# Half of the attention scores streamed over 64 columns: exchanged key halves, three transposes, and a new order of loads

## The chip, the cores and the metric

The kernel runs on one core of a Trainium2 chip. The metric is the device time of one execution, in microseconds. Before the change it was 646.65 us, the median of three runs (646.60, 646.65 and 646.69).

## What is computed

The reference chains three layers. A linear attention with a decay per channel and a bonus for the current token comes first, over 2 batches, 8 heads, 768 tokens and 48 channels per head. Its output, 1536 tokens of 384 features, goes through a feed-forward layer with ELU (384 to 2048 to 384) and then through four dense experts with ReLU (384 to 1024 to 384), weighted by normalised probabilities.

```python
def _attn_ref(r, k, v, w, u):
    for t in range(S):
        cur = np.einsum('bhd,bhe->bhde', u[None] * kt, vt)
        y[:, :, t] = np.einsum('bhd,bhde->bhe', rt, state + cur)
        state = wt[:, :, :, None] * state + np.einsum('bhd,bhe->bhde', kt, vt)

x = attn_out.transpose(0, 2, 1, 3).reshape(1536, 384)
h = x @ w_in
x = np.where(h > 0, h, np.exp(np.minimum(h, 0)) - 1) @ w_out
p = domain_probs / (domain_probs.sum(-1, keepdims=True) + 1e-9)
out = sum(p[:, e:e+1] * (np.maximum(x @ w1[e], 0) @ w2[e]) for e in range(4))
```

## The kernel before

The 1536 tokens are 12 chunks of 128 (6 per batch, the batches taken in turn), numbered 0 to 11. In a chunk, tokens are held in the order 63 down to 0, then 64 to 127: the first half is turned round, and decays are taken from the middle of the chunk. Heads go in four pairs `p`; of a pair, head `o` = 0 lies in partitions 0 to 47 and head `o` = 1 in 64 to 111.

For each chunk the attention does this. VectorE forms running products of the decays (`products`, `inverses`), scales k and r with them (`scale_k` L892, `scale_r` L906), and TensorE multiplies them to scores, keys by queries (`scores`, L1183 to 1202). GpSimd puts the bonus on the diagonal of `att` (`bonus_terms` L519 to 528, `bonus_diagonal` L531 to 538), VectorE copies the scores over it where the mask allows (`mask_scores` L909 to 922), and TensorE multiplies with the old state (`old_values` L1279) and with v (`values_even` L1291, `values_odd` L1295 and L1299). For the state, k has to be turned: VectorE transposes it in blocks of 32 x 32 (`turn_blocks` L895 to 900), SP writes the blocks to DRAM and reads them back as `kt_sb` (`move_blocks`, L455 and L460), and TensorE multiplies them with v (`update`, L1233). Chunks 0 and 1 go another way (scores at L1196, turned on TensorE); chunks 2 to 9 are turned as said, and 10 and 11, the last of each batch, need no update.

Scores of keys in the second half (64 to 127) and queries in the first (0 to 63) are always masked. Before the change they are computed all the same: for each pair and head two matmuls, one for each half of the keys, each over all 128 queries. A matmul of fp32 is two records in the trace. With 48 rows and 64 columns of weights the four (o, half) of a pair lie in four quadrants of the array.

The attention doesn't run by itself. TensorE's order is written out by hand as steps `n` of the first feed-forward layer: a step is an up-projection of one slice of 128 hidden features for one tile of tokens, and a down-projection of the step but one before (`LAG` = 2). Tiles have 256, 256, 512 and 512 tokens, 16 slices each. `SCORES` says in which step a chunk's scores stand: chunk c at 4c up to 8, then every third step, at the end of the step; its values follow two steps later. Other operations have their step relative to that (`PRODUCTS` -4, `HALF_INVERSES` -3, `SCALE_K` -2, `SCALE_R` -1, turned k in the step of `scale_k`, but for chunks 3, 4 and 8 one later, behind `scale_r`: `LATE_TURNS`). VectorE and ScalarE serve the feed-forward layer in the same queues. ScalarE takes relu and exp of the hidden values (L763, L765), VectorE finishes the ELU in PSUM (L997), ScalarE rounds it (`hi_g` L771), VectorE takes the rest (`lo_g` L1003), since every product is made in three passes of high and low parts.

Weights are split likewise: in the first tile ScalarE copies each slice rounded to `w_hi` (L723 and L728, in halves from slice 6, where `HI_BETWEEN` says: slice 12 in step 9, 13 in 10, 14 in 11, 15 in 12 and 13), and GpSimd (`lo_w` L547) or VectorE (L967) takes the rest to `w_lo`. GpSimd's queue is w_lo halves, with the bonus terms of chunks 2 and 3 and their diagonals between.

All loads here are on SP's queue, in the order of its program: decays and k, r of chunks 0 and 1, constants, v of 0 and 1, slices 0 to 7, `load_rkw(2)`, `load_tok(2)`, u, slices 8 and 9, `load_rkw(3)`, `load_tok(3)`, slices 10 to 15, probabilities; then for c = 4 to 11 `load_rkw(c)` (k, r and decays by channel, L442), `load_tok(c)` (r, k and v by token, L449) and `move_blocks(c - 2)`. `load_rkw(c)` waits for the values of chunk c-3, `move_blocks` for the turned blocks, its reads also for the landing of its write. Three buffers each hold the chunks in turn.

After 165 us only the feed-forward layers run. The change doesn't touch them.

## Time and profile before

| | |
|---|---|
| median of 3 runs | 646.65 us (646.60 to 646.69) |
| the profiled execution | 646.8 us |
| its span | 645.0 us |
| instructions | 13796 |
| TensorE matmul busy | 638.5 us (99%) |
| TensorE weight load busy | 591.7 us (92%) |
| VectorE busy | 419.4 us (65%) |
| ScalarE busy | 237.2 us (37%) |
| GpSimd busy | 296.1 us (46%) |

The profile is one execution. Its time of 646.8 us lies 0.15 us above the median, and 1.8 us of it lie around the span. Times in the trace count from the span's start. PE is TensorE's matmuls, PEld its weight loads, DVE VectorE, ACT ScalarE, POOL GpSimd, SPq the DMA issues of SP. A row of the timeline merges neighbours of one kind: start, time from the first start to the last end, line, operation, what it writes and reads, how many. In brackets stands the idle time in front of it and what ended it. Matmuls overlap in the array, so the distance from start to start is what one costs, not its duration.

### The profile page before, as it was taken

The page shows a single profiled execution, that of the slowest core. Times are in us where ns is not written, and L with a number is a line of the kernel's source. Part 1 is how long each engine was busy: PE and PEld are TensorE (multiplying, and loading weights), DVE is VectorE, ACT ScalarE, POOL GpSimd, SP SyncE. Part 2 cuts the span into 40 slices and gives each one's busy share as a digit, 9 for nine tenths or more (in the row PEclk, how much of TensorE's full clock was granted, in tenths as well). Part 3 has the DMA queues.
Part 4 walks back from the last instruction along what each step waited for, and adds up shares of the span by engine and source line. Part 5 has one row for each costly group of instructions (what it writes and reads, how often), then busy time and mean ns, then how long its engine had stood idle before and what let it go on. Part 6 is the DMA issues. An engine that isn't in the chain of part 4 may idle for free.

```text
span 645.0 us, 13796 instructions
## 1 busy us (share of the span) xinstructions
PE 638.5 (99%) x5046; PEld 591.7 (92%) x5046; DVE 419.4 (65%) x786; ACT 237.2 (37%) x557; POOL 296.1 (46%) x370
## 2 busy tenths in 40 slices
PE   8999999999999999999999999999999999999998
PEld 5998999877788888999999999999999999999997
DVE  7889999874357666565555555565656565656564
ACT  4785555655445554222222222222222222222221
POOL 5897424420799899994029900019900018000000
PEclk9999999999999999999999999999999999999999
DMA  9954454300000233000013100012100011001011
GB/s 328 404 186 137 138 182 162 124 14 1 1 2 1 73 98 100 27 2 0 1 50 99 50 1 0 1 49 99 50 1 0 0 50 50 0 1 49 0 50 50
DMA packets 19043, 42.34 MB, mean 66 GB/s; under 512 B 2608, under 2 KB 8752, under 8 KB 18992
## 3 DMA queue, kind: packets, MB, share of 16 engines
q1 hardware_dynamic: 18704, 41.23, 18.7%
q8 instruction: 36, 0.59, 0.4%
q10 hardware_dynamic: 288, 0.39, 0.2%
q14 instruction: 15, 0.12, 0.1%
HBM read 37.16 MB, written 4.46 MB: 65 GB/s over the span
## 4 chain that ended last, share of the span: by engine, by line
PE 91%; DVE 3%; POOL 3%; issue 1%; DMA 0%; ACT 0%; DVEq 0%; POOLq 0%
PE bank L1366 29%; PE bank L1367 29%; PE bank L1368 29%; POOL w_lo L547 3%; PE bank L1200 1%; PE bank L1279 1%; PE bank L1291 1%; DVE fr L864 1%; DMA rkw<-rkw_dram 0%; DVE fr L883 0%; PE bank L1233 0%; PE bank L1299 0%; PE bank L1295 0%; DVE w_lo L967 0%; DVE rkw L906 0%
## 5 line engine op out<-in xcount | busy, mean ns | idle before, releaser
L1366 PE MATMUL bank<-x_lo,w_hi 128*128 128x256 f32 (+2 forms) x416 | 138.0, 332 | 0.6 <-POOL w_lo L547 0.5
L1367 PE MATMUL bank<-x_hi,w_lo 128*128 128x256 f32 (+2 forms) x416 | 135.2, 325 | 0.0
L1368 PE MATMUL bank<-x_hi,w_hi 128*128 128x256 f32 (+2 forms) x416 | 135.2, 325 | 0.0
L1367 PE MATMUL bank<-w_hi,g_lo 128*128 128x384 f32 x384 | 129.6, 337 | 0.0
L1368 PE MATMUL bank<-w_hi,g_hi 128*128 128x384 f32 x384 | 129.3, 337 | 0.0
L1366 PE MATMUL bank<-w_lo,g_hi 128*128 128x384 f32 x384 | 129.0, 336 | 0.0
L827 ACT ACTIVATE g_hi<-bank 128x512 fp32r<-128x512 f32 x96 | 57.5, 599 | 144.3 <-DVE bank L1053 122.4
L1366 PEld LDWEIGHTS bank<-x_lo,w_hi 128*128 128x128 f32 x416 | 78.2, 188 | 10.4 <-issue 2.5
L1368 PEld LDWEIGHTS bank<-x_hi,w_hi 128*128 128x128 f32 x416 | 78.2, 188 | 7.5
L1367 PEld LDWEIGHTS bank<-x_hi,w_lo 128*128 128x128 f32 x416 | 78.3, 188 | 7.1
L1046 DVE TENSOR_TENSOR u_sum<-p_copy,bank 128x256 f32<-128x256 f32 x56 | 23.6, 421 | 92.1 <-ACT p_copy L751 91.3
L559 POOL TENSOR_TENSOR raw<-raw 128x128 f32<-128x128 f32 x16 | 7.5, 469 | 160.5 <-DMA raw<-w_dram 160.5
L1366 PEld LDWEIGHTS bank<-w_lo,g_hi 128*128 128x128 f32 x384 | 72.2, 188 | 0.0
L1368 PEld LDWEIGHTS bank<-w_hi,g_hi 128*128 128x128 f32 x384 | 72.1, 188 | 0.0
L1367 PEld LDWEIGHTS bank<-w_hi,g_lo 128*128 128x128 f32 x384 | 72.0, 188 | 0.0
L1135 DVE SCALAR_TENSOR_TENSOR g_lo<-bank,g_hi 128x512 fp32r<-128x512 f32 x96 | 65.9, 686 | 7.1 <-ACT g_hi L827 6.8
L751 ACT COPY p_copy<-bank 128x256 f32<-128x256 f32 x56 | 21.0, 375 | 134.4 <-PE bank L1368 134.2
L1366 PE MATMUL bank<-g_lo,w_hi 128*128 128x256 f32 (+1 forms) x192 | 65.1, 339 | 0.0
L1368 PE MATMUL bank<-g_hi,w_hi 128*128 128x256 f32 (+1 forms) x192 | 64.9, 338 | 0.0
L1367 PE MATMUL bank<-g_hi,w_lo 128*128 128x256 f32 (+1 forms) x192 | 64.7, 337 | 0.0
L571 POOL TENSOR_TENSOR w_lo<-raw,w_hi 128x768 fp32r<-128x768 f32 x32 | 58.6, 1855 | 0.0
L1051 DVE TENSOR_TENSOR bank<-p_copy,bank 128x256 f32<-128x256 f32 x56 | 24.0, 429 | 51.4 <-PE bank L1368 51.4
(134 smaller groups left out, 1272.6 us busy)
## 6 DMA issues: line engine op xcount, KB each, us to landing
raw<-w_dram SPq DMA_DIRECT2D x48, 384.0 KB, 3.7
rkw<-rkw_dram SPq DMA_DIRECT2D x10, 772.5 KB, 4.6
tok<-tok_dram SPq DMA_DIRECT2D x10, 576.0 KB, 6.8
k_blocks_dram<-k_blocks SPq DMA_DIRECT2D x8, 256.0 KB, 4.3
kt_sb<-k_blocks_dram SPq DMA_DIRECT2D x32, 64.0 KB, 2.0
out_dram<-acc SPq DMA_DIRECT2D x10, 192.0 KB, 1.9
rkw<-rkw_dram SPq DMA_DIRECT2D x2, 512.0 KB, 4.2
rkw<-rkw_dram SPq DMA_DIRECT2D x2, 260.5 KB, 3.4
```

Source lines behind the costliest of these rows:

```text
L547: pool.tensor_tensor(w_lo[:, n, part], raw[:, n, part], w_hi[:, n, part].bitcast(F32), ALU.subtract).then_inc(s_wq, 1)
L559: pool.tensor_tensor(s1, a21, a22, ALU.add).then_inc(s_ws, 1)
L571: pool.tensor_tensor(w_lo[:, slot, :], raw[:, slot, :], w_hi[:, slot, :].bitcast(F32), ALU.subtract).then_inc(s_w, 1)
L751: act.copy(p_copy[:, 0, :], bank[6][:, 0:QUARTER]).then_inc(s_pc, 1)
L827: act.activation(g2[0][:, p % 2 * 2 + o, :], bank[o][:, :], ACT.Relu).then_inc(s_gh, 1)
L864: dve.tensor_tensor_scan(fr[:, 0:SCAN], rkw[c % DEEP][:, 2 * NRK:2 * NRK + SCAN], reset[:, :], 0.0, ALU.mult, ALU.add).then_inc(s_f, 1)
L1046: dve.tensor_tensor(u2, p1, p6, ALU.add).then_inc(s_u2, 1)
L1051: dve.tensor_tensor(c11, p1, c11, ALU.add).then_inc(s_c, 1)
L1135: dve.scalar_tensor_tensor(out=g2[1][:, r, :], in0=bank[o][:, :], scalar=0.0, in1=g2[0][:, r, :].bitcast(F32), op0=ALU.max, op1=ALU.subtra ...
L1366: pe.matmul(out, wh, ml, start=start, stop=False, skip_group_check=shared)
L1367: pe.matmul(out, wl, mh, start=False, stop=False, skip_group_check=shared)
L1368: return pe.matmul(out, wh, mh, start=False, stop=stop, skip_group_check=shared)
```

## The change

- `scores`, chunks 2 to 11: of each head, the matmul of the early keys streams all 128 queries, that of the late keys only the 64 late ones. For pairs 0 and 1 (`exchanged`) the late keys are written to partitions 0 to 63 of the bank and the early ones to 64 to 127; for pairs 2 and 3 as before. The order goes by two pairs, 0 and 2, then 1 and 3, and the pairs lie in the bank as 0, 2, 1, 3 (`place`). Still 16 matmuls.
- All that meets the exchanged keys follows. By-token rows of heads 0 to 3 are loaded with halves exchanged: `load_tok` is three DMAs (64 rows, 64 rows, 128 rows, each of 3 x 192 columns) and not one. Turned k: `turn_blocks` is three transposes of 128, 128 and 256 columns. The diagonal is three selects of 256, 256 and 512 elements, not two of 512. A second mask with exchanged halves is loaded by two small DMAs behind `load_tok(3)`, and `mask_scores` uses both masks, on two blocks of 256 columns. It waits for all three selects where the first half waited for one, and in chunk 2 for the mask. The sums of the bonus are written in another order of heads.
- `move_blocks` becomes `write_blocks` and `read_blocks`, and both stand ahead of `load_tok`. Slices 12 and 13 stand between the write and the reads of chunk 2, slices 14 and 15 behind `load_tok(4)`.

```diff
             def load_rkw(c):
                 need(sp, s_py, c - DEEP + 1)
-                need(sp, s_kb, c - DEEP + 1 - FIRST)
+                need(sp, s_kb, 3 * (c - DEEP + 1 - FIRST))
...
-                sp.dma_start(tok[c % DEEP][:, :], tok_d[c]).then_inc(s_tok[c % DEEP], 16)
...
+                sp.dma_start(columns(here[0:HALF, :], 0), columns(there[HALF:CH, :], 0)).then_inc(s_tok[c % DEEP], 16)
+                sp.dma_start(columns(here[HALF:CH, :], 0), columns(there[0:HALF, :], 0)).then_inc(s_tok[c % DEEP], 16)
+                sp.dma_start(columns(here[:, :], DM // 2), columns(there, DM // 2)).then_inc(s_tok[c % DEEP], 16)
...
-            sp.dma_start(const[:, :], const_d).then_inc(s_const, 16)
+            sp.dma_start(const[:, P:3 * P], const_d[:, C_MASK:C_MASK + 2 * P]).then_inc(s_const, 16)
...
-            load_slices(10, 11, 12, 13, 14, 15)
+            for rows, others in ((slice(0, HALF), slice(HALF, CH)), (slice(HALF, CH), slice(0, HALF))):
+                sp.dma_start(const[rows, 0:P], const_d[others, C_MASK:C_MASK + P]).then_inc(s_exchanged, 16)
+            load_slices(10, 11)
             sp.dma_start(probs[:, :, :], probs_d).then_inc(s_probs, 16)
             for c in range(4, NC):
                 load_rkw(c)
+                write_blocks(c - 2)
+                if c == 4:
+                    load_slices(12, 13)
+                read_blocks(c - 2)
                 load_tok(c)
-                move_blocks(c - 2)
+                if c == 4:
+                    load_slices(14, 15)
...
-                for o in range(2):
-                    pool.affine_select(att[:, o, :, :], heads[:, o, :].unsqueeze(2).broadcast_to([P, PAIRS, CH]),
...
+                diagonal(0, 0, HALF, HALF)
+                diagonal(0, HALF, HALF, 0)
+                diagonal(1, 0, CH, 0)
...
-                dve.transpose(k_blocks[:, :, :].rearrange("q t (a j) -> q t a j", a=PAIRS),
-                              raw_k(c).rearrange("q (a t i) -> q t a i", a=PAIRS, i=STRIP)).then_inc(s_kb, 1)
+                strips = raw_k(c).rearrange("q (a t i) -> q t a i", a=PAIRS, i=STRIP)
+                turned = k_blocks[:, :, :].rearrange("q t (a j) -> q t a j", a=PAIRS)
+                dve.transpose(turned[:, 0:2, 0:2, :], strips[:, 2:4, 0:2, :]).then_inc(s_kb, 1)
+                dve.transpose(turned[:, 2:4, 0:2, :], strips[:, 0:2, 0:2, :]).then_inc(s_kb, 1)
+                dve.transpose(turned[:, :, 2:4, :], strips[:, :, 2:4, :]).then_inc(s_kb, 1)
...
-                    dve.wait_ge(s_diag, diagonal_done(c) - 1 + o)
-                    dve.copy_predicated(att[:, o, :, :], masks.bitcast(I32), found).then_inc(s_att, 1)
+                    dve.wait_ge(s_diag, diagonal_done(c))
+                    found = banks["x"][o][:, :].rearrange("p (a t) -> p a t", a=PAIRS // 2)
+                    dve.copy_predicated(att[:, o, :, :].rearrange("p (a b) t -> p a (b t)", b=2),
+                                        both_masks.unsqueeze(1).broadcast_to([P, PAIRS // 2, 2 * CH]).bitcast(I32),
+                                        found).then_inc(s_att, 1)
...
+                def block(p, o, later, first, count):
+
+                    rows, at = slice(64 * o, 64 * o + D), HALF * (later != exchanged(p))
+                    out = place(c, p) * CH + first
+                    return pe.matmul(banks["x"][o][at:at + HALF, out:out + count],
+                                     k[rows, p * CH + HALF * later:p * CH + HALF * later + HALF],
+                                     q[rows, p * CH + first:p * CH + first + count], start=True, stop=True)
+
+                for p in range(PAIRS // 2):
+                    for one in (p, p + PAIRS // 2):
+                        for o in range(2):
+                            block(one, o, 0, 0, CH)
+                        for o in range(2):
+                            ins = block(one, o, 1, HALF, HALF)
```

## Rows read from the trace of the kernel before

**Rows 1.** The page: TensorE's busy time, and the chain by engine.
```profile
PE 638.5 (99%) x5046; PEld 591.7 (92%) x5046; DVE 419.4 (65%) x786; ACT 237.2 (37%) x557; POOL 296.1 (46%) x370
...
PE 91%; DVE 3%; POOL 3%; issue 1%; DMA 0%; ACT 0%; DVEq 0%; POOLq 0%
```

**Rows 2.** Timeline of TensorE at two waits: start, time, line, what, [idle before <-releaser].
```profile
37.21 0.36 PE L1366 MATMUL bank<-x_lo,w_hi 128*128 128x256 f32 x1 [0.51 <-POOL w_lo L547]
...
61.45 0.34 PE L1200 MATMUL bank<-rkw 48*64 48x128 f32 x4 [0.44 <-DVE rkw L906]
```

**Rows 3.** Windows by stage: length, busy time by engine, granted clock, DMA share, GB/s.
```profile
17.00:37.00 20.00, 19.70 (x218) 18.95 (x213) 17.67 (x39) 15.82 (x45) 18.15 (x23) 1.00 0.96 376
...
61.00:73.50 12.50, 12.03 (x193) 11.46 (x192) 11.80 (x25) 7.16 (x24) 4.39 (x6) 1.00 0.47 160
```

**Rows 4.** Timeline of VectorE: turned k of chunk 5, scaled r of chunks 5, 6, 7.
```profile
70.97 0.71 DVE L899 STREAM_TRANSPOSE k_blocks<-rkw 128x512 f32<-128x512 f32 x1
71.60 0.70 DVE L931 TENSOR_TENSOR st<-bank,st 64x192 f32<-64x192 f32 x2
...
72.80 0.69 DVE L906 TENSOR_TENSOR rkw<-rkw,fr 128x512 f32<-128x512 f32 x1
...
84.53 0.69 DVE L906 TENSOR_TENSOR rkw<-rkw,fr 128x512 f32<-128x512 f32 x1
...
96.27 0.69 DVE L906 TENSOR_TENSOR rkw<-rkw,fr 128x512 f32<-128x512 f32 x1
```

**Rows 5.** Timeline of TensorE: the first scores of chunks 5, 6 and 7.
```profile
73.55 0.34 PE L1200 MATMUL bank<-rkw 48*64 48x128 f32 x4
...
85.49 0.34 PE L1200 MATMUL bank<-rkw 48*64 48x128 f32 x4
...
97.44 0.34 PE L1200 MATMUL bank<-rkw 48*64 48x128 f32 x4
```

**Rows 6.** Timeline of ScalarE: its waits on TensorE in chunks 7 and 8.
```profile
94.35 0.39 ACT L763 ACTIVATE neg<-bank 128x256 f32<-128x256 f32 x1 [0.68 <-PE bank L1368]
...
106.31 0.39 ACT L763 ACTIVATE neg<-bank 128x256 f32<-128x256 f32 x1 [0.90 <-PE bank L1368]
```

**Rows 7.** Timeline of TensorE: tiled matmuls, and what follows the scores of chunk 8.
```profile
16.46 0.67 PE L1225 MATMUL bank<-tok,kt_sb 128*64 128x48 f32 x16
...
104.49 0.52 PE L1233 MATMUL bank<-tok,kt_sb 128*32 128x48 f32 x32
...
110.40 1.10 PE L1200 MATMUL bank<-rkw 48*64 48x128 f32 x32
...
111.43 0.50 PE L1366 MATMUL bank<-x_lo,w_hi 128*128 128x512 f32 x1
```

**Rows 8.** VectorE by line and form, 61 to 97 us: busy, mean ns | idle before.
```profile
L1003 DVE TENSOR_TENSOR g_lo<-bank,g_hi 128x256 fp32r<-128x256 f32 x13 | 5.3, 409 | 1.3 <-ACT g_hi L771 1.3
...
L950 DVE TENSOR_TENSOR x_lo<-bank,x_hi 128x384 fp32r<-128x384 f32 x2 | 1.1, 549 | 0.0
...
L873 DVE RECIPROCAL inv_end<-fr 128x8 f32<-128x8 f32 x3 | 0.6, 207 | 0.1
```

**Rows 9.** Timeline of GpSimd and VectorE: diagonal and mask of chunk 5.
```profile
74.83 1.22 POOL L536 TENSOR_SCALAR_AFFINE_SELECT att<-bonus_sb 128x512 f32<-128x512 f32 x2 [7.59 <-DVE bonus_sb L938]
...
77.87 1.36 DVE L922 COPY_PREDICATED att<-const,bank 128x512 f32<-128x512 int32 x2
```

**Rows 10.** Timeline of SP and ScalarE, the landings of L455, DMA issues of slices.
```profile
32.74 0.33 SPq L455 DMA_DIRECT2D k_blocks_dram<-k_blocks  x1
37.39 1.86 SPq L460 DMA_DIRECT2D kt_sb<-k_blocks_dram  x4
...
45.74 0.91 ACT L728 CAST w_hi<-raw 128x384 fp32r<-128x384 f32 x2
...
DMA to landing us min/median/max: 2.0/4.3/5.8
...
raw<-w_dram SPq DMA_DIRECT2D x48, 384.0 KB, 3.7
```

More of the change, by code:

```diff
@@ L295, in bass_linear_attention_elu_ffn_dense_experts, with tok_landed, exchanged, place @@
         s_dr = sem("s_dr")
-        mask = const[:, C_MASK:C_MASK + P]
-        ident = const[:, C_ID:C_ID + P]
+        both_masks = const[:, 0:2 * P]
+        mask = const[:, P:2 * P]
+        ident = const[:, 2 * P:3 * P]
         def landed(eng, sems, c):
             eng.wait_ge(sems[c % DEEP], 16 * (c // DEEP + 1))
+        def tok_landed(eng, c):
+            parts = 3 * (c // DEEP + 1) - (2 if c % DEEP < FIRST else 0)
+            eng.wait_ge(s_tok[c % DEEP], 16 * parts)
+        def exchanged(p):
+            return p < PAIRS // 2
+        def place(c, p):
+            return p if c < FIRST else p % 2 * 2 + p // 2
         def raw_q(c):
@@ L937, in bonus @@
                 bonus_done(dve, c - 2)
-                dve.tensor_reduce(bonus_sb[:, c % 2, :], tok[c % DEEP][:, 0:DM].rearrange("p (h d) -> p h d", h=H),
+                dve.tensor_reduce(bonus_sb[:, c % 2, :].rearrange("p (b o a) -> p b a o", b=2, o=2),
+                                  tok[c % DEEP][:, 0:DM].rearrange("p (b a o d) -> p b a o d", b=2, o=2, d=D),
                                   AX.X, ALU.add).then_inc(s_bon, 1)
```

63 lines of the change are left out of this document (35 added, 28 removed).

## The prediction

> **What bounds the kernel now.** I read the shares of busy time first: TensorE is busy 99% of a 645.0 us span, and the chain that ended last is 91% TensorE [rows 1]. From the windows view on, the question is therefore not whether TensorE bounds the whole, but where another engine sets its pace for a while, since only the attention part (17 to 165 us) is touched. The view of waits sent me to two such places in TensorE's timeline: at 37.21 us, 0.51 us on GpSimd's `w_lo` (slice 9), and at 61.45 us, 0.44 us on the vector engine's scaled r in front of the scores of chunk 4 [rows 2]. The windows by stage show why the second matters: from 61 to 73.5 us VectorE is busy 11.80 of 12.50 us, nearly as full as TensorE, while DMA is at 0.47; from 17 to 37 us it is DMA that is full, 0.96; the granted clock is 1.00 in both [rows 3].
>
> Next I set the ends of the scaled r beside the starts of the scores that need it. Chunk 5: r ends at 72.80+0.69 = 73.49, scores start at 73.55. Chunk 6: 85.22 and 85.49. Chunk 7: 96.96 and 97.44 [rows 4, 5]. The handover takes some 0.06 us (chunk 5, where TensorE had waited), so the slack is 0, 0.21, 0.42 us. VectorE goes round in 11.73 us per chunk (72.80, 84.53, 96.27), TensorE in 11.94 and 11.95. That VectorE isn't carried along by TensorE in this stretch, the scalar engine shows: its one wait on TensorE per chunk grows from 0.68 to 0.90 us [rows 6], which it would not if both went at one pace. So from about 46 us (where I place the start, after the GpSimd wait at 37 and the update of chunk 2) to 97 us there are two loops side by side, VectorE with ScalarE at 11.73 and TensorE at 11.95 us per chunk, and VectorE's lead at the end is 0.42 us. Behind that, with tiles of 512 tokens, TensorE alone is the bound.
>
> **The scores.** One chunk has 16 matmuls, 32 records, in four quadrants of the array. From the row, starts are (1.10-0.27)/31 = 26.8 ns apart, or 107 ns per pass of 128 columns in one quadrant; from the first score to the next matmul of another line it is 111.43-110.40 = 1.03 us [rows 7]. Eight passes per quadrant make 0.86 us of it. The change leaves the number of matmuls, but half of them stream 64 columns, and since the halves of pairs 0 and 1 are exchanged each quadrant gets four long and four short passes. Nothing before has a 64-column pass. From below: half of 107, 53 ns. From above, no gain at all, 107 ns. The nearest row is that of L1225, weights of 64 columns as here and 48 columns streamed: (0.67-0.22)/15 = 30 ns for two tiles, 60 ns per pass; with weights of 32 columns the same 48 take (0.52-0.21)/31 x4 = 40 ns [rows 7]. So the load of 64 weight columns, not the stream, seems to set some 58 to 60 ns. I take 58: 4 x (107-58) = 0.20 us saved per chunk. All of it on TensorE is 10 x 0.20 = 2.0 us. Whether four quadrants really work independently when the passes are unequal is open; if matmuls start strictly in order, a short pass can wait behind a long one of another quadrant, and counting out the order loses 0.05 us a chunk. That is kept in the range.
>
> The Trainium skill, page "TensorE: Matmul & The Clock Gate", section "Wait — 56ns, not 53.3ns?", says that starts of matmuls are never closer than about 25 ns, however few columns they have. The 26.8 ns of the row are just above that, and by the rule this edit would save at most 32 x 1.8 ns a chunk. The trace doesn't agree for matmuls in separate tiles: L1233 starts one every (0.52-0.21)/31 = 10 ns [rows 7]. The case is a rival below all the same.
>
> **VectorE.** `turn_blocks` becomes three transposes of 128, 128 and 256 columns for one of 512. The elements are the same, so two fixed costs come on top. Operations of 256 and 384 columns take 409 and 549 ns, so 128 columns are 0.14 us; a transpose of 512 is followed 71.60-70.97 = 0.63 us later, and 0.63-4x0.14 leaves 0.07 fixed [rows 4, 8]. From below: 0 (hidden in its neighbours, or in a wait). From above: the 207 ns that an operation of 8 columns takes from start to end [rows 8], if the parts don't overlap at all. I take 0.10 each, since the row of 0.07 is the nearest and a wait or a semaphore may add a little: d = 0.20 us per turn. In the queue of VectorE, the turn of chunk 3 stands before the scaled r of chunk 4, that of chunk 4 before the r of chunk 5, and those of 5, 6 and 7 before their own: five turns in the self-paced stretch. (The turn of chunk 2 lies ahead of the GpSimd wait, those of 8 and 9 where TensorE is the bound.) There, VectorE falls back by 5 x 0.20 = 1.0 us.
>
> The Trainium skill, page "VectorE: DVE Perf Modes", section "The TRN2 errata", speaks against this split too: each operation pays a fixed cost, 58 cycles for a source in SBUF. As an estimate from that page it is 2 x 0.06 = 0.12 us a turn and 0.6 us for five turns instead of 1.0.
>
> `mask_scores` reads the same 512 columns twice; it now waits for all diagonals before the first half. Behind it in the queue stand an ELU and the factors of the next chunk, and the values of the chunk wait for it. But GpSimd's diagonal ends at 74.83+1.22 = 76.05, a third instruction adds 0.1, and the mask starts at 77.87 [rows 9]: nothing. The reduction writes its 8 sums in another order, same elements: nothing. The extra wait for the exchanged mask falls on chunk 2 only, with its load issued in the first 20 us.
>
> **Queues.** By-token loads become three DMAs, two more issues of about 0.5 us on SP each for chunks 2 to 11, in pieces of 768 bytes. From chunk 4 on they stand behind the moves of turned k, used a chunk later by GpSimd: nothing on the path. In front they cost SP 1 us twice before slices 8 and 10, while DMA is a full queue anyhow [rows 3]. Then SP's order is: write of chunk 2 (after its turn, 32.74 now), slices 12 and 13, four reads, tok 4, slices 14 and 15. The reads were issued at 37.39, 4.6 us behind the write; such a write lands in 2.0 us at best and 5.8 at worst [rows 10], and with four slices of 384 KB gone from the full stretch I take 2.0. Then, at some 0.47 us an issue, as the four reads show, and 3.7 us from issue to landing for a slice [rows 10]: slices 12 and 13 at 33.9 + 3.7 = 37.6; reads issued by 35.2 + 1.9 = 37.1, tok 4 by 38.5, slices 14 and 15 at 39.4 + 3.7 = 43.1. If the write again takes 4.6 us, this is 45.7. ScalarE copies slice 14 at 45.74 [rows 10], and 12 and 13 one and two steps ahead of that. So the cover is 2.6 us, and hardly any at the bad end; if it went, the scalar engine's queue would stop, with its `g_hi` copies behind, and VectorE with it. For later chunks turned k no longer stands behind tok in the DMA queues, which gives its update more slack; no update waits for it now, so nothing is gained.
>
> GpSimd gets one more select in front of `w_lo` halves 9 to 12, 0.1 us; the wait at 37.21 lies before it. That wait takes the saving of chunk 2's scores whole, since TensorE then only waits longer.
>
> **The sum.** Scores of chunk 7 start when VectorE delivers: 96.96+0.06+1.0 = 98.02, against 97.44 now, +0.58 us. The savings of chunks 2 to 6 are all spent in waits there. From chunk 7 on TensorE is the bound again: five chunks (7 to 11) save 5 x 0.20 = 1.0. Together -0.42 us. Against the profiled execution (645.0 us span, 646.8 in all) that is 646.4; the median of the runs is 646.65, and from there I forecast **646.2 us**. In terms of d the change is -1.42 + 5d: at d = 0 it gives 645.2, at the upper bound, 0.40, 647.2.
>
> **The rivals.**
> - TensorE takes the full gain (12%): the two added transposes hide in VectorE's waits on the scalar engine (some 0.9 us per chunk, 12.50-11.80 and the like [rows 3]). Chunks 4 to 11 save 8 x 0.20: -1.6, 645.0. Against it: those waits are answers to VectorE's own ELU and move with it.
> - The short matmuls gain nothing (8%), be it by a floor on starts or because the weight load holds each quadrant. The scores stay at 1.03 us, only the loss of VectorE stays: +0.58, 647.2. Against it: matmuls in separate tiles start 10 ns apart, and the 48-column passes of L1225 take 60 ns, not 107 [rows 7]. (The Trainium skill's 25 ns between starts, cited above, would be such a floor.)
> - Slower (8%): slices 14 and 15 behind the by-token load come late. The copy of slice 14 stands at 45.74 in ScalarE's queue, and from there to 97 us each late microsecond passes to VectorE and on to the scores. With the forecast's -0.4 it makes the kernel slower at all from a landing at 46.2 us, and measurably from 47.5; at 48.2 it gives 646.2 + 2.4 = 648.6. For it: three DMAs with six times as many pieces, and a step that waits for the turn. Against: 2.6 us of cover.
> - The order makes no difference that counts (2%): the compiled quadrants behave as before and the turns cost nothing, 646.6.
>
> **Chances.** The forecast's case has 70%: its own range, with d from 0 to 0.40, is 645.2 to 647.2, and 0.05 us a chunk less on the scores adds 0.25. The range 645.2 to 647.3 takes in the floor rival as well and leaves out the full gain, 0.2 below it, and the late slices. About 0.2%, 1.3 us, is what a measurement of this kernel can tell from no change. Faster than 645.35 is the full gain and a small part of my own case: 0.16. Slower than 647.95: 0.08. The same: 0.76.
>
> **What would show it.** Right: scores of a chunk take 0.83 us from first to next line; TensorE waits on scaled r at the scores of chunks 4 to 7, in all over 1 us; chunk 7's scores start near 98.0; chunk 11's near 150.7. Wrong: no such waits (the turns are free), an unchanged 1.03 us for the scores, or ScalarE waiting on a weight slice between 39 and 50 us. The prediction falls with d above all: each 0.1 us of it is worth 0.5 us.

## The result: 648.49 us, slower by 0.3%, and the profile after

The changed kernel takes 648.49 us in the median of 9 runs (648.34 to 649.29), the kernel before 646.60 us (646.55 to 646.75, 9 runs). The ratio is 1.0031, 95% interval 1.0022 to 1.0039: slower, by 1.9 us. The forecast was 646.2 us and the range ended at 647.3. The profiled execution is the slowest of the nine, 649.29 us with a span of 647.6 us, 0.8 above the median; against the span before, 645.0, it shows 2.6 us to be explained. The difference between the medians is 1.9 us; no execution near the median was traced, so the waits below may be up to 0.8 us longer than in a typical one.

The line numbers have moved: scores L1200 are L1251, passes of the steps L1366 to L1368 are L1425 to L1427, scaled r L906 is L947, turned k L899 is L939 to L941, ScalarE's copy of a slice L728 is L766. From the page of the changed kernel, busy time and chain (as [rows 1]):

```profile
PE 637.0 (98%) x5046; PEld 590.2 (91%) x5046; DVE 421.3 (65%) x802; ACT 237.0 (37%) x557; POOL 296.7 (46%) x380
...
PE 81%; DVE 9%; SPq 3%; ACT 3%; issue 2%; DMA 1%; POOL 0%; DVEq 0%; ACTq 0%; POOLq 0%
```

TensorE had 91% of the chain and has 81%. SP and DMA, with nothing to speak of before, now hold 4% of it, and the windows view says where. Its columns are those of [rows 3]; the last two are the DMA share and the rate in GB/s.

```profile
17.00:37.00 20.00, 17.83 (x172) 17.09 (x173) 16.00 (x36) 12.85 (x35) 16.50 (x23) 1.00 0.89 274
61.00:73.50 12.50, 11.70 (x189) 10.90 (x188) 11.84 (x26) 7.27 (x25) 6.88 (x11) 1.00 0.36 115
```

From 17 to 37 us TensorE does 17.83 us of work instead of 19.70, and DMA moves 274 GB/s instead of 376. The timelines of ScalarE, then of TensorE, in that stretch:

```profile
32.33 0.51 ACT L766 CAST w_hi<-raw 128x384 fp32r<-128x384 f32 x1 [2.74 <-DMA raw<-w_dram]
```
```profile
33.63 0.39 PE L1425 MATMUL bank<-g_lo,w_hi 128*128 128x256 f32 x1 [1.36 <-DVE g_lo L1050]
...
36.83 0.39 PE L1425 MATMUL bank<-g_lo,w_hi 128*128 128x256 f32 x1 [0.81 <-DVE g_lo L1050]
...
38.09 0.90 PE L1251 MATMUL bank<-rkw 48*64 48x128 f32 x32
...
38.92 0.39 PE L1425 MATMUL bank<-x_lo,w_hi 128*128 128x256 f32 x1
```

ScalarE stands 2.74 us for weight slice 10. Its `g_hi` stands behind the copy in its queue, VectorE's `g_lo` waits for that, and TensorE for `g_lo`: 1.36 and 0.81 us. The scores of chunk 2 start at 38.09 us; before, they started at 35.60. The chain that ended last, from 19 us on, names what made the slice late:

```profile
19.41 2.39 SPq L515
...
21.84 0.79 SPq L515
...
22.67 9.64 DMA raw<-w_dram
...
32.33 0.02 ACT w_hi L766
```

And SP's own timeline ahead of that:

```profile
13.71 3.00 SPq L444 DMA_DIRECT2D raw<-w_dram  x2
16.75 0.43 SPq L457 DMA_DIRECT2D rkw<-rkw_dram  x1
17.36 0.70 SPq L468 DMA_DIRECT2D tok<-tok_dram  x1
18.11 0.61 SPq L469 DMA_DIRECT2D tok<-tok_dram  x1
18.76 0.61 SPq L470 DMA_DIRECT2D tok<-tok_dram  x1
19.41 3.22 SPq L515 DMA_DIRECT2D const<-const_dram  x2
22.67 1.93 SPq L444 DMA_DIRECT2D raw<-w_dram  x2
```

In the kernel before, SP and ScalarE had this:

```profile
10.59 0.93 SPq L429 DMA_DIRECT2D raw<-w_dram  x2
...
17.59 2.81 SPq L429 DMA_DIRECT2D raw<-w_dram  x6
```
```profile
29.72 0.50 ACT L728 CAST w_hi<-raw 128x384 fp32r<-128x384 f32 x1
```

SP issues the two small mask loads for 3.22 us, slices 8 and 9 for 3.00 and slices 10 and 11 for 1.93 us, where two slices took 0.93 us before: it is held up. Slices 8 and 9 are issued 3.1 us later than before, slice 10 5.1 us later, at 22.67 and not at 17.59. By the landings slice 10 arrives at 32.31 us, before at 28.52, where its copy began at 29.72. So there were 1.2 us of cover (the time between the landing of a transfer and its first use), and the delay was 3.8.

The delay stays. Starts of the scores in us, chunks 2 to 11 (first L1200 or L1251 of each, from TensorE's timeline):

```
chunk      2      3      4      5      6      7       8       9      10      11
before  35.60  48.08  61.45  73.55  85.49  97.44  110.40  125.35  141.35  150.96
after   38.09  50.49  63.96  76.45  88.47 100.48  113.25  128.58  144.38  153.79
later    2.49   2.41   2.51   2.90   2.98   3.04    2.85    3.23    3.03    2.83
```

2.4 to 2.5 us are lost before chunk 3. All that the new scores save (ten times 0.20 us) is spent again. A step that kept its saving would be 0.20 us shorter than before. From chunk 4 to 5 it is 0.39 us longer (12.49 against 12.10), from 8 to 9 0.38 (15.33 against 14.95), and from 5 to 6 and 6 to 7 it takes 12.02 us instead of 11.95; from 7 to 8 and behind 9 the saving is there.

### The profile page after: what moved, and what is told of

It is laid out like the page before. It is cut to its first block, busy times and chain, and to the rows that moved or that the text cites. A ratio compares the mean times of both kernels' runs of the same rounds, so it can differ in the third digit from the quotient of the medians.

```text
span 647.6 us, 13845 instructions
## 1 busy us (share of the span) xinstructions
PE 637.0 (98%) x5046; PEld 590.2 (91%) x5046; DVE 421.3 (65%) x802; ACT 237.0 (37%) x557; POOL 296.7 (46%) x380
## 4 chain that ended last, share of the span: by engine, by line
PE 81%; DVE 9%; SPq 3%; ACT 3%; issue 2%; DMA 1%; POOL 0%; DVEq 0%; ACTq 0%; POOLq 0%
PE bank L1425 27%; PE bank L1426 26%; PE bank L1427 26%; DVE bank L1044 2%; DVE fr L902 2%; DMA raw<-w_dram 1%; DVE att L966 1%; SPq L444 1%; DVE rkw L930 1%; ACT neg L801 1%; ACT neg L803 1%; ACT alpha L728 1%; ACT g_hi L809 1%; DVE fr L921 1%; DVE st L977 0%
## 5 line engine op out<-in xcount | busy, mean ns | idle before, releaser
L1425 PE MATMUL bank<-x_lo,w_hi 128*128 128x256 f32 (+2 forms) x416 | 138.1, 332 | 0.5 <-POOL w_lo L585 0.4
L1427 PE MATMUL bank<-x_hi,w_hi 128*128 128x256 f32 (+2 forms) x416 | 135.2, 325 | 0.0
L1427 PE MATMUL bank<-w_hi,g_hi 128*128 128x384 f32 x384 | 129.3, 337 | 0.0
L1425 PE MATMUL bank<-w_lo,g_hi 128*128 128x384 f32 x384 | 129.0, 336 | 0.0
L1425 PEld LDWEIGHTS bank<-x_lo,w_hi 128*128 128x128 f32 x416 | 78.2, 188 | 9.6 <-issue 1.0
L1427 PEld LDWEIGHTS bank<-x_hi,w_hi 128*128 128x128 f32 x416 | 78.2, 188 | 7.5
L1425 PEld LDWEIGHTS bank<-w_lo,g_hi 128*128 128x128 f32 x384 | 72.1, 188 | 0.0
L1427 PEld LDWEIGHTS bank<-w_hi,g_hi 128*128 128x128 f32 x384 | 72.0, 188 | 0.0
L1425 PE MATMUL bank<-g_lo,w_hi 128*128 128x256 f32 (+1 forms) x192 | 65.5, 341 | 2.8 <-DVE g_lo L1050 2.2
L1427 PE MATMUL bank<-g_hi,w_hi 128*128 128x256 f32 (+1 forms) x192 | 64.9, 338 | 0.0
L609 POOL TENSOR_TENSOR w_lo<-raw,w_hi 128x768 fp32r<-128x768 f32 x32 | 58.5, 1852 | 0.0
```

Source lines behind the costliest of these rows:

```text
L609: pool.tensor_tensor(w_lo[:, slot, :], raw[:, slot, :], w_hi[:, slot, :].bitcast(F32), ALU.subtract).then_inc(s_w, 1)
L1425: pe.matmul(out, wh, ml, start=start, stop=False, skip_group_check=shared)
L1427: return pe.matmul(out, wh, mh, start=False, stop=stop, skip_group_check=shared)
```

## The experiments

Two questions: what held up slice 10, and where the saved 2 us went. Every kernel ran beside the kernel before on the same chip. Given are the median and the ratio to the kernel before with its 95% interval.

### Slices 10 and 11 first

```diff
             load_slices(8, 9)
+            load_slices(10, 11)
             load_rkw(3)
             load_tok(3)
...
-            load_slices(10, 11)
             sp.dma_start(probs[:, :, :], probs_d).then_inc(s_probs, 16)
```

> The changed kernel with one thing altered: weight slices 10 and 11 are issued ahead of chunk 3's loads instead of behind them and the two small mask DMAs. Theory A (the time was lost because slice 10 landed 3.8 us later than before, behind by-token loads cut into 768-byte pieces, so that ScalarE stood 2.74 us for it): slice 10 lands near 28.5 us again, ScalarE's wait of 2.74 us for it goes, the scores of chunk 2 start near 35.7 instead of 38.1, and the time falls by 1.9 to 2.4 us, to 646.2 to 646.8. Rival B (the time was lost in the chunks, on VectorE: two more transposes in each turn of k and a scan that lasts 0.14 us longer): the first chunks come earlier but the end hardly does, 648.0 to 648.5. Rival C (chunk 3's loads now arrive late instead): a wait of ScalarE or GpSimd for chunk 3's tok of 1 us or more, 647.5 to 648.5.

646.76 us, ratio to the kernel before 1.0003 (0.9994 to 1.0012). ScalarE's timeline again:

```profile
29.62 0.50 ACT L766 CAST w_hi<-raw 128x384 fp32r<-128x384 f32 x1
```

The wait is gone, chunk 2's scores start at 35.51. One line moved gives back 1.7 us, and the kernel can't be told from the one before. The load by token of chunk 3 now lands at 32.3 us instead of 31.1, and GpSimd wants it at 47 only: rival C is out. Rival B is out as the cause of the loss, but what it describes is there: from chunk 5 on its scores start 0.35 to 0.8 us behind those of the kernel before.

### The pieces alone

In the kernel before, a load by token as three DMAs, for which all its readers wait:

```diff
-                sp.dma_start(tok[c % DEEP][:, :], tok_d[c]).then_inc(s_tok[c % DEEP], 16)
+                sp.dma_start(columns(here[0:HALF, :], 0), columns(there[0:HALF, :], 0)).then_inc(s_tok[c % DEEP], 16)
+                sp.dma_start(columns(here[HALF:CH, :], 0), columns(there[HALF:CH, :], 0)).then_inc(s_tok[c % DEEP], 16)
+                sp.dma_start(columns(here[:, :], DM // 2), columns(there, DM // 2)).then_inc(s_tok[c % DEEP], 16)
```

> The kernel before with one part of the change alone: each load by token goes as three DMAs with 768-byte pieces for r and k's first and second halves of the columns, with nothing exchanged, and those who read it wait for all three. The order of all loads is that of before, slices 10 to 15 follow chunk 3's loads, and the two small mask DMAs are not there. Theory A (the 768-byte pieces hold up the slices): slice 10 lands 3 to 4 us later than before (31.5 to 32.5 instead of 28.52), ScalarE waits for it, and the kernel is 1.8 to 2.5 us slower than before, 648.4 to 649.1. If the mask DMAs carry half of it, slice 10 lands near 30.5 and the time is 647.2 to 647.8. Rival B (VectorE in the chunks): 646.5 to 646.8, since no work of VectorE is added here.

650.56 us (649.10 to 656.78), ratio 1.0072 (1.0044 to 1.0100). With no mask load and nothing exchanged, slice 10 lands at 31.9 us, 3.4 of the 3.8 us late. ScalarE waits 1.37 us for it, and chunk 2's scores start at 37.10, 1.5 us late where the changed kernel had 2.5. The rest of the 3.9 us comes later and is more than I gave the pieces: in the order of before, in which turned k stands behind the loads by token, TensorE's update of chunk 2 comes to wait as well (and another, for 0.6 us, between the scores of chunks 6 and 7):

```profile
46.03 0.55 PE L1244 MATMUL bank<-tok,kt_sb 128*32 128x48 f32 x32 [1.71 <-DMA kt_sb<-k_blocks_dram]
```

The changed kernel, with the same pieces and the new order of the moves, has no such wait.

### Pieces twice as large

In the kernel before, three DMAs again, but r, k and v whole:

```diff
-                sp.dma_start(tok[c % DEEP][:, :], tok_d[c]).then_inc(s_tok[c % DEEP], 16)
+                for i in range(3):
+                    part = slice(i * DM, (i + 1) * DM)
+                    sp.dma_start(tok[c % DEEP][:, part], tok_d[c][:, part]).then_inc(s_tok[c % DEEP], 16)
```

> The kernel before with each load by token as three DMAs of r, k and v whole: as many DMAs and issues on SP as in the changed kernel, but pieces of 1536 bytes instead of 768. Theory (the small pieces fill the queues): a third of the way or less, slice 10 lands by 29.5 us, ScalarE waits less than 0.3 us for it, and the time is 646.5 to 647.0. Rival (three issues on SP for one and their share of the queue, whatever the pieces): slice 10 lands at 31 us or later and the time is that of the kernel with the 768-byte pieces, above 648.

647.14 us, 1.0005 (0.9996 to 1.0014), 0.3 us over the 646.85 of its group. Slice 10 lands at 28.5 us, as before, and is copied at 29.66. There are as many DMAs for a load as in the change, and nothing is lost for the slices: it isn't their number but their form. The form differs in two ways, though. The pieces are of 1536 bytes and not of 768, and all three DMAs cover 128 rows, where two of the change's three cover 64. No run separates these two. In the changed kernel the DMA records of chunk 3's 768-byte pieces, in the order of their start, have medians of 45 and 72 ns for the two quarters that should be the DMAs of 64 rows and of 54 and 46 for those of the third, so the pieces are dear in both; which piece belongs to which DMA the records don't tell. The windows view from 18 to 30 us, where DMA is full, for the kernel before, the changed kernel, the pieces alone, and this one:

```profile
18.00:30.00 12.00, 12.00 (x129) 11.68 (x128) 10.42 (x23) 9.10 (x25) 10.59 (x14) 1.00 1.02 401
```
```profile
18.00:30.00 12.00, 12.00 (x129) 11.67 (x128) 10.44 (x24) 8.90 (x24) 10.59 (x14) 1.00 1.07 300
```
```profile
18.00:30.00 12.00, 11.98 (x128) 11.58 (x127) 10.42 (x22) 8.47 (x23) 10.45 (x15) 1.00 1.07 318
```
```profile
18.00:30.00 12.00, 12.00 (x128) 11.68 (x128) 10.42 (x23) 9.15 (x25) 10.59 (x14) 1.00 1.04 392
```

The share is over 1 in all four: by it the changed kernel's DMA is as full as ever, but it moves 300 GB/s instead of 401. Over 12 us that is 1.2 MB less, or 3.0 us at the old rate, most of the 3.8 us by which slice 10 is late. With 1536-byte pieces it is 392.

### The halves exchanged in DRAM

```diff
-                sp.dma_start(columns(here[0:HALF, :], 0), columns(there[HALF:CH, :], 0)).then_inc(s_tok[c % DEEP], 16)
-                sp.dma_start(columns(here[HALF:CH, :], 0), columns(there[0:HALF, :], 0)).then_inc(s_tok[c % DEEP], 16)
-                sp.dma_start(columns(here[:, :], DM // 2), columns(there, DM // 2)).then_inc(s_tok[c % DEEP], 16)
+                sp.dma_start(tok[c % DEEP][:, :], tok_d[c]).then_inc(s_tok[c % DEEP], 16)
...
+    tok[FIRST:, :, :, 0:DM // 2] = np.roll(tok[FIRST:, :, :, 0:DM // 2], HALF, axis=1)
```

> The changed kernel with r and k by token already exchanged in DRAM for the late chunks, so that a load by token is one DMA in pieces of 4608 bytes again; the order of all loads, with slices 10 and 11 behind chunk 3's loads and the mask DMAs, is that of the changed kernel. Theory A (the pieces, not the place of slice 10): slice 10 lands near 29 us, ScalarE's wait of 2.74 us is gone, and the time is that of the run with the slices first, 646.5 to 646.9. Rival (the two mask DMAs and the order are at fault, and the run with the slices first only stepped around them): slice 10 lands at 30.5 us or later, ScalarE waits 0.8 us or more for it, and the time is 647.3 to 648.5.

646.87 us, 1.0002 (0.9993 to 1.0011): as with the slices first. Slice 10 lands at 28.5, the copy starts at 29.70, though the mask loads and the order are those of the change. SP issues the two mask loads in 1.19 us here instead of 3.22:

```profile
17.58 1.19 SPq L508 DMA_DIRECT2D const<-const_dram  x2
```

They are slow only where the queues hold the small pieces. The mask loads and the order don't cost this time by themselves.

### The order alone

The kernel before with turned k in front of the loads by token, slices 12 and 13 behind its write, 14 and 15 behind tok 4.

```diff
                 load_rkw(c)
+                write_blocks(c - 2)
+                if c == 4:
+                    load_slices(12, 13)
+                read_blocks(c - 2)
                 load_tok(c)
-                move_blocks(c - 2)
+                if c == 4:
+                    load_slices(14, 15)
```

> The kernel before with the new order of SP's queue alone: turned k is moved in front of the loads by token, slices 12 and 13 behind its write, 14 and 15 behind tok 4. By the prediction nothing is won or lost: slice 14 lands near 43 us, copied near 45.7, and the time is 646.5 to 646.8. If the slices come late (46.2 us or later), up to 648.6. If turned k's earlier arrival is worth something, under 646.4.

646.71 us, 1.0000 (0.9991 to 1.0009). Slice 14 lands at 42.6 us, where the prediction worked out 43.1. That is near by luck in part: it was issued at 36.94 and not at 39.4, and took 5.6 us and not 3.7.

### The scores alone

In the kernel before, with `block` as in the change but the pairs in their old places. The masks, the diagonal, turned k and the by-token loads stay unexchanged, so for pairs 0 and 1 this kernel leaves out what would make its result the attention; it only measures the time.

```diff
-                        for half in range(2):
-                            keys = slice(p * CH + HALF * half, p * CH + HALF * half + HALF)
-                            ins = pe.matmul(banks["x"][o][HALF * half:HALF * half + HALF, cols], k[rows, keys],
-                                            q[rows, cols], start=True, stop=True)
...
+                for p in range(PAIRS // 2):
+                    for one in (p, p + PAIRS // 2):
+                        for o in range(2):
+                            block(one, o, 0, 0, CH)
+                        for o in range(2):
+                            ins = block(one, o, 1, HALF, HALF)
```

> The kernel before with the new scores alone, in the late chunks: two pairs write their key halves to exchanged partitions, and the masked quarter is not computed. Everything behind it (mask, diagonal, k turned, r and k by token) stays unexchanged, so what it computes for these two pairs is not the attention of the reference; the work on all engines but TensorE is that of before. It measures the saving where VectorE keeps its old load. By the prediction's formula with no added turn cost: -1.42 us, 645.2, scores of chunk 7 at 97.0 and TensorE waiting for scaled r there. If VectorE's own pace is slower than the 11.73 us that I read (it may have been carried along by TensorE), less: -1.0, 645.6. If it is TensorE that paces all ten chunks: -2.0, 644.6.

645.65 us, 0.9985 (0.9977 to 0.9994): faster, by 1.05 us. The scores take 0.83 us. TensorE's timeline, chunks 5 to 8:

```profile
73.45 0.90 PE L1204 MATMUL bank<-rkw 48*64 48x128 f32 x32
...
85.19 0.90 PE L1204 MATMUL bank<-rkw 48*64 48x128 f32 x32
...
97.27 0.90 PE L1204 MATMUL bank<-rkw 48*64 48x128 f32 x32
...
110.11 0.90 PE L1204 MATMUL bank<-rkw 48*64 48x128 f32 x32
```

From chunk 5 to 6 it is 11.74 us, the old 11.95 less the saving, and no wait for scaled r: VectorE with its old load keeps up, as its 11.73 us had said. From 6 to 7 it is 12.08. The 0.3 us over are one wait of the weight load at 92.34 us for turned k (0.40, `kt_sb`), which in the order of before stands behind the loads by token. Without it the run would be at -1.35, next to the -1.42 of the formula, but not by its parts: behind chunk 7 the gain is 0.78 us (chunk 7 starts 0.17 us earlier than before, chunk 11 0.75, and its own 0.20), not 1.0. From chunk 8 to 9 only 0.06 us are gained.

### Three transposes, and three selects

In the kernel before:

```diff
-                dve.transpose(k_blocks[:, :, :].rearrange("q t (a j) -> q t a j", a=PAIRS),
-                              raw_k(c).rearrange("q (a t i) -> q t a i", a=PAIRS, i=STRIP)).then_inc(s_kb, 1)
+                dve.transpose(turned[:, 0:2, 0:2, :], strips[:, 0:2, 0:2, :]).then_inc(s_kb, 1)
+                dve.transpose(turned[:, 2:4, 0:2, :], strips[:, 2:4, 0:2, :]).then_inc(s_kb, 1)
+                dve.transpose(turned[:, :, 2:4, :], strips[:, :, 2:4, :]).then_inc(s_kb, 1)
```

> The kernel before with k turned in three transposes (halves not exchanged) and all else as before. The trace of the changed kernel has them at 0.76 us against 0.64 us for one, so 0.12 us a turn. Where VectorE paces the chunks (five turns by the prediction's count) that is +0.6 us, 647.2; with the prediction's 0.20 us a turn it would be 1.0 us, 647.6; if all ten turns count, 1.2 us, 647.8; if VectorE has room after all, nothing, 646.6. The scan should keep its 1.53 us if the diagonal is what lengthens it, and go to 1.67 us if the transposes are.

646.96 us, 1.0006 (0.9997 to 1.0015): a third of a microsecond, not told from nothing. The profiled execution took 647.31. The scores of chunk 5 start 0.43 us later than before, 0.34 of which are there from chunk 2 on, but 6 and 7 come 11.95 us apart: TensorE sets the pace there. The scan keeps its 1.53 us.

```diff
-                for o in range(2):
+                for o, first, count in ((0, 0, HALF), (0, HALF, HALF), (1, 0, CH)):
...
-                    dve.wait_ge(s_diag, diagonal_done(c) - 1 + o)
+                    dve.wait_ge(s_diag, diagonal_done(c))
```

> The kernel before with the diagonal put in by three selects (256, 256 and 512 wide) instead of two of 512, both masks waiting for all three, nothing exchanged. The prediction priced this at nothing on the path: 646.6, with GpSimd 0.1 us longer in a chunk. The new theory has it shift GpSimd's products against VectorE's scan, which lasts 1.67 us in the changed kernel instead of 1.53: then the scan is 0.1 to 0.15 us longer here too, and with five chunks paced by VectorE the time is 0.5 to 0.75 us longer, 647.1 to 647.4.

646.85 us, 1.0004 (0.9995 to 1.0013). GpSimd, then VectorE, in chunk 6:

```profile
86.71 1.37 POOL L536 TENSOR_SCALAR_AFFINE_SELECT att<-bonus_sb 128x256 f32<-128x256 f32 x3 [7.33 <-DVE bonus_sb L939]
88.05 2.08 POOL L524 TENSOR_TENSOR tok<-tok 128x192 f32<-128x192 f32 x2
```
```profile
88.06 1.68 DVE L865 TENSOR_TENSOR_SCAN fr<-rkw,reset 128x520 f32<-128x520 f32 x1
```

The third select makes the diagonal 0.15 us longer. GpSimd's products of r and k then begin 0.02 us ahead of VectorE's scan and no longer 0.16, and the scan takes 1.68 us instead of 1.53. The mechanism is as expected, the price is not: here TensorE hides it. In the kernel with the slices first both additions are together, 0.12 (transposes) and 0.14 (scan), and the scores are shorter: there it is VectorE that TensorE waits for.

Why does a smaller lead cost more? The single instructions show it. In the kernel before, GpSimd, then VectorE, in chunk 4 and in chunk 5:

```profile
64.04 1.52 POOL L524 TENSOR_TENSOR tok<-tok 128x192 f32<-128x192 f32 x1
```
```profile
63.90 1.27 DVE L864 TENSOR_TENSOR_SCAN fr<-rkw,reset 128x520 f32<-128x520 f32 x1
```
```profile
76.02 0.60 POOL L524 TENSOR_TENSOR tok<-tok 128x192 f32<-128x192 f32 x1
```
```profile
76.18 1.53 DVE L864 TENSOR_TENSOR_SCAN fr<-rkw,reset 128x520 f32<-128x520 f32 x1
```

Alone the scan takes 1.23 us and the product 0.60 (half of the pair's time where nothing is beside it). The one that begins first nearly keeps its time, and the other is longer. What the scan loses is what is left of GpSimd's operation when it begins, less some 0.13 us: 0.60 - 0.16 = 0.44 left and 0.30 lost, 0.58 left and 0.45 lost. This holds for a select as well: in chunk 4 a select has 0.18 us left and the scan takes 1.27 us; with three selects it has 0.32 left and the scan takes 1.41. So by these rows one of the two stands while the other works. (The 0.13 us is read from these runs; why it is there stays open.)

### The products out of the scan's way

In the kernel with the slices first, GpSimd's products run one diagonal earlier:

```diff
+            bonus_terms(4)
...
-            for c in range(4, NC):
+            for c in range(5, NC):
                 bonus_terms(c)
-                bonus_diagonal(c)
+                bonus_diagonal(c - 1)
+            bonus_diagonal(NC - 1)
```

> The changed kernel with slices 10 and 11 first, and with GpSimd's products of r, k and u for a chunk run ahead of the diagonal of the chunk before it instead of behind it (from chunk 4 on). In the traces so far those products start together with VectorE's scan, which then takes 1.5 to 1.7 us, against 1.23 us where GpSimd does nothing beside it. Theory (VectorE's own work sets 12.02 us a chunk where TensorE needs 11.74): the scan takes 1.25 us, chunks 5 to 7 come 11.74 to 11.85 us apart, and the kernel is 0.9 to 1.4 us faster than with the slices first, 645.4 to 645.9, faster than the kernel before. Rival (the contention only moves to other operations of VectorE): 12.0 us a chunk and 646.6 to 646.9. Rival (chunks 4 to 7 are paced by something else, such as ScalarE's handovers): the scan is short, and the time is still 646.6 to 646.9.

646.79 us, 0.9999 (0.9990 to 1.0008); the profiled execution took 647.08. VectorE in chunk 6, with the slices first and then with the products early:

```profile
88.64 1.69 DVE L902 TENSOR_TENSOR_SCAN fr<-rkw,reset 128x520 f32<-128x520 f32 x1
```
```profile
88.88 1.23 DVE L904 TENSOR_TENSOR_SCAN fr<-rkw,reset 128x520 f32<-128x520 f32 x1
```

TensorE's scores of chunks 5 to 7 in the same two kernels:

```profile
73.98 0.90 PE L1251 MATMUL bank<-rkw 48*64 48x128 f32 x32
...
86.01 0.90 PE L1251 MATMUL bank<-rkw 48*64 48x128 f32 x32 [0.22 <-DVE rkw L947]
...
98.02 0.90 PE L1251 MATMUL bank<-rkw 48*64 48x128 f32 x32 [0.19 <-DVE rkw L947]
```
```profile
74.83 0.90 PE L1253 MATMUL bank<-rkw 48*64 48x128 f32 x32 [0.27 <-DVE rkw L949]
...
86.58 0.90 PE L1253 MATMUL bank<-rkw 48*64 48x128 f32 x32
...
98.33 0.90 PE L1253 MATMUL bank<-rkw 48*64 48x128 f32 x32
```

The scan is 0.46 us shorter, the waits for scaled r are gone, and the chunks come 11.75 us apart instead of 12.02: those 12.02 us were VectorE's own pace. The whole is not faster, though, because chunk 5 starts 0.85 us later. Some 0.4 of that are there from chunk 2 on (35.93 us against 35.51), where nothing was changed; the kernel with three transposes in before shows the same start, 35.94. It is the same contention, decided by a hair. With the slices first, one of chunk 2's two scans of 260 columns begins 0.02 us before a `w_lo` of GpSimd and takes 0.70 us; here it begins 0.01 us after it. VectorE in the two kernels:

```profile
27.41 0.70 DVE L921 TENSOR_TENSOR_SCAN fr<-rkw,inv_end 128x260 f32<-128x260 f32 x1
```
```profile
27.38 1.14 DVE L923 TENSOR_TENSOR_SCAN fr<-rkw,inv_end 128x260 f32<-128x260 f32 x1
```

Together with three transposes that makes TensorE late. With one transpose (the kernel with three selects, 1.15 us for this scan) the scores of chunk 2 start at 35.51 all the same. Which of the two begins first may differ from one execution to the next, and only one of each kernel was traced. For the other 0.45 there is a reason: GpSimd does the products of two chunks in a row at 58.5 to 63.9 us and the diagonal of chunk 4 only behind them, and VectorE's mask waits 0.32 us for it. So the first theory holds for the pace, and the time that it gave was wrong.

> The kernel before with that new order of GpSimd alone. TensorE paces chunks 5 to 7 there (11.94 us apart, no wait at the scores), so VectorE's shorter scan should win only what TensorE waits for scaled r at chunk 4's scores and little else: 0 to 0.5 us, 646.1 to 646.6. If it wins as much as in the changed kernel, the scan and not the change's load on VectorE is what that run measures.

The same order of GpSimd in the kernel before: 646.87 us, 1.0000 (0.9991 to 1.0009). The pace stays 11.95 us. VectorE isn't the bound there, and the order by itself is worth nothing.

With the halves exchanged in DRAM and the products early from chunk 6 on only:

```diff
-            for c in range(4, NC):
+            bonus_terms(4)
+            bonus_diagonal(4)
+            bonus_terms(5)
+            for c in range(6, NC):
                 bonus_terms(c)
-                bonus_diagonal(c)
+                bonus_diagonal(c - 1)
...
```

> The kernel with r and k by token exchanged in DRAM (one DMA a load), and GpSimd's products ahead of the diagonal of the chunk before from chunk 6 on only, so that the diagonal of chunk 4 is not put off as it was with the change from chunk 4 on (it ended at 66.2 us there, and VectorE's mask waited 0.3 us). Theory: chunks 4 and 5 start as with the slices first (61.5 and 74.0), chunks 6 and 7 come 11.75 us apart (scan 1.23 us), so the scores of chunk 7 start near 97.5 instead of 98.0 and the end is 0.5 us earlier than in the kernel with the halves exchanged in DRAM: 646.2 to 646.4, 0.05% faster than the kernel before, which these rounds can hardly tell. Rival (what VectorE wins is lost again behind chunk 7, in the steps of 512 tokens): 646.7 to 646.9.

646.68 us, 0.9997 (0.9988 to 1.0006), from 645.96 to 647.16. The profiled execution, 647.12, is from the upper end. It starts chunk 2 at 36.05, again 0.45 late (the scan at 27.49 takes 1.15 us), and chunk 5 at 74.87, since the products now stretch VectorE's scaled k. Chunks 6 and 7 follow 11.74 and 11.75 us apart. GpSimd and VectorE ahead of chunk 5:

```profile
71.00 1.61 POOL L548 TENSOR_TENSOR tok<-tok 128x192 f32<-128x192 f32 x2 [2.97 <-DMA tok<-tok_dram]
```
```profile
71.06 1.08 DVE L927 TENSOR_TENSOR rkw<-rkw,fr 128x512 f32<-128x512 f32 x1
```

Scaled k is 0.68 us without such company. Part of the contention moves, and when the products run depends on when tok 6 lands. No version that computes the reference was measurably faster than the kernel before.

### The exchange in the writes

One transpose again, the halves exchanged on the way to DRAM, on top of the kernel with by-token halves laid out there:

```diff
-                sp.dma_start(scratch, k_blocks[:, :, :]).then_inc(s_written, 16)
+                half = PAIRS // 2 * STRIP
+                sp.dma_start(scratch[:, 0:2, 0:half], k_blocks[:, 2:4, 0:half]).then_inc(s_written, 16)
+                sp.dma_start(scratch[:, 2:4, 0:half], k_blocks[:, 0:2, 0:half]).then_inc(s_written, 16)
+                sp.dma_start(scratch[:, :, half:], k_blocks[:, :, half:]).then_inc(s_written, 16)
...
```

> The kernel with r and k by token exchanged in DRAM, and with k turned in one transpose again: the halves of two pairs are exchanged in the write to DRAM, which becomes three DMAs (pieces of 256 bytes for a part). VectorE then carries only the longer scan (0.14 us a chunk). Theory: each turn costs 0.63 instead of 0.76 us, chunks 4 to 7 come 11.9 instead of 12.02 us apart, and the end is 0.5 to 0.6 us earlier than with the slices first: 646.0 to 646.3. If the three writes land too late for the update (a wait of TensorE for the turned k, kt_sb), it loses what the wait is long. If TensorE rather than VectorE set those 12.02 us, the time stays 646.6 to 646.9.

647.51 us, 1.0015 (1.0006 to 1.0023): slower. The second case that it names came true, at chunk 4's update:

```profile
70.76 0.55 PE L1285 MATMUL bank<-tok,kt_sb 128*32 128x48 f32 x32 [1.73 <-DMA kt_sb<-k_blocks_dram]
```

Chunks 5 to 7 come 11.75 us apart behind that, but VectorE had been handed a lead of 1.7 us, so it doesn't show whether one transpose would have been enough.

## Why the prediction was wrong, step by step

**Queues: the step that failed.** "In front they cost SP 1 us twice before slices 8 and 10, while DMA is a full queue anyhow": from the full queue I read that an issue more is free. It is the reverse. A full queue is where the bytes per microsecond count, and I had counted issues and put the price of the pieces at nothing, without a row: the kernel before moves none of 768 bytes. The rate fell from 401 to 300 GB/s, slice 10 came 3.8 us late on 1.2 us of cover, and 1.7 of the 1.9 us of the result are that (undone by the slices first and by the halves in DRAM; with the pieces alone slice 10 is as late). The issues were mis-sized too: the "1 us twice" became 3.1 us ahead of slice 8 and, with the mask loads, 5.1 in all ahead of slice 10. The rows for a warning were at hand: the stretch from 17 to 37 us at 0.96 [rows 3], and the landing of every slice beside its copy. I worked out that margin for slices 12 to 15, which the change moves in the text, and not for 10 and 11, which it moves only in time.

**The rival "slower"** had the right mechanism, its price per late microsecond and its place in ScalarE's queue, but the wrong slice, and so 8%. Slice 14 landed at 47.22 us and was copied at 47.54, 0.3 us of cover with everything 2.5 us later.

**The scores:** 38.92 - 38.09 = 0.83 us, as worked out, in the other chunks too. The sum fits four quadrants that don't disturb each other; the single passes weren't measured. The rival of no gain would have left 1.03 us. The floor of 25 ns between starts (the Trainium skill, "TensorE: Matmul & The Clock Gate", section "Wait — 56ns, not 53.3ns?") doesn't hold for matmuls in separate tiles: they now start (0.90 - 0.27)/31 us apart, 20 ns, and those of L1233 10 ns [rows 7].

**Turned k:** d is 0.12 us, not 0.20. From VectorE's timeline of the changed kernel:

```profile
85.77 0.31 DVE L939 STREAM_TRANSPOSE k_blocks<-rkw 128x128 f32<-128x128 f32 x1
86.01 0.27 DVE L940 STREAM_TRANSPOSE k_blocks<-rkw 128x128 f32<-128x128 f32 x1
86.20 0.40 DVE L941 STREAM_TRANSPOSE k_blocks<-rkw 128x256 f32<-128x256 f32 x1
86.53 0.70 DVE L977 TENSOR_TENSOR st<-bank,st 64x192 f32<-64x192 f32 x2
```

86.53 - 85.77 = 0.76 us for three, 0.63 for one. That is 0.13 here and 0.12 in other chunks. The row that I had (0.07 fixed) was better than the 0.10 that I made of it. (The "some 0.9 us" of waits in the rival of the full gain is a slip as well: 12.50 - 11.80 is 0.70.) The Trainium skill's 58 cycles each ("VectorE: DVE Perf Modes", section "The TRN2 errata"), 0.12 us by the estimate, is what these rows show.

**The diagonal, "nothing":** wrong by its side effect. The cover was asked for the mask that waits for it, and that holds. What starts behind it in GpSimd's own queue wasn't asked: the products, begun 0.15 us later, have more left when the scan begins and hold it up 0.14 us more. So a chunk costs VectorE 12.02 us against 11.73, 0.29 more (0.12 and 0.14 are 0.26 of it), where I had 0.20.

**Chunk 7's scores:** forecast 98.02, and with the slices first 98.02. That is luck in part, from errors that cancel: 0.29 us a chunk instead of 0.20, but not five times, since chunk 4's scores start at 61.47, hardly later than before (61.45), and the turn of chunk 3 doesn't count. The mechanism, VectorE's slack of 0.42 us used up and TensorE waiting for scaled r, is there in the rows above.

**Behind chunk 7:** forecast -1.0 us over five chunks, measured -0.43 with the slices first (chunk 7 0.58 us later than before, chunk 11 0.35, less its own 0.20). Chunk 8 to 9 is 15.35 us instead of 14.95. "TensorE alone is the bound" was too simple there: VectorE's backlog reaches into the steps of 512 tokens. In the kernel with the slices first:

```profile
118.83 0.50 PE L1425 MATMUL bank<-g_lo,w_hi 128*128 128x512 f32 x1 [0.32 <-DVE x_lo L1055]
```

The sum, with the queue's 1.7 us taken away, would then have been +0.1 where I had -0.4: inside its range, and "the same". Left open is why the three DMAs of the change are so dear when all DMA engines are at work, and which of their two sides it is, the 768-byte pieces or the DMAs of 64 rows. The runs show that three DMAs of 128 rows and 1536 bytes are not, and where the time goes, but not why.

## What to carry to other kernels

When an edit cuts a transfer into smaller pieces, ask for the bytes per microsecond of the stretch in which it runs, and for the landing of everything queued behind it, moved or not, beside the time at which it is wanted. A DMA share near 1 means no room, not no cost. And where an instruction grows on an engine with room to spare, ask also what it pushes: two engines may now want to work at the same moment that used not to, and then it counts which of them begins first.

## What the runs showed of the hardware

A 768-byte piece takes 36 ns in the quieter stretch from 40 to 60 us and 52 to 55 ns (medians of the DMA records, the pieces alone) from 10 to 40 us, where the queues are full. A 1536-byte piece takes 65 to 66 ns in both (the kernel with r, k and v whole), but 76 ns beside the small ones (the 128 pieces of the load of u, the pieces alone). SP's issue of two small loads goes from 1.19 to 3.22 us when the queues hold such pieces.

VectorE's scan of 520 columns takes 1.23 us alone. A GpSimd operation that is already at work holds it up: 1.53 us where the products have begun 0.16 us earlier, 1.68 us where they have begun 0.02 us earlier, 1.41 us behind a select with 0.32 us left. Where the scan is ahead of the product GpSimd pays: 1.52 us for a product of 0.60. A scan of 260 columns takes 0.70 or 1.14 us, and between these two lies a change of 0.03 us in which of the engines is ahead.
